# Fused bucket attention and expert layer on one core: one weight chunk more in the attention phase, and small shifts of work between engines

## The reference

```python
q_bits = (einsum('bhsd,dk->bhsk', q, proj) > 0)      # 6 bits, the same for k
mask = q_bucket[:, :, :, None] == k_bucket[:, :, None, :]
scores = where(mask, q @ k.T / sqrt(64), -1e9)
attn_out = softmax(scores) @ v
x = attn_out.transpose(0, 2, 1, 3).reshape(2, 768, 512)
logits = x @ w_gate                                   # 8 experts
local_gate = sigmoid(x @ w_local)
# along s: e = argmax(logits) if s == 0 or local_gate < 0.5, else the previous row's e
h = maximum(x @ w1[e], 0)                             # 512 -> 1024
out = softmax(logits)[e] * (h @ w2[e])                # 1024 -> 512
```

## Time and profile before

| what | value |
|---|---|
| median of 3 runs | 481.82 us (478.69 to 482.27) |
| the profiled execution: time | 481.82 us |
| the profiled execution: span of the trace | 480.0 us |
| mean granted clock of TensorE | 0.982 |
| busy: PE, POOL, ACT, DVE | 453.1, 337.9, 299.2, 260.7 us |

### The profile page before, as it was taken

The page is one execution under the profiler, slowest core; times in us unless marked ns, Lnnn a source line. Parts: engine busy times, 40 slices in busy tenths (PEclk is TensorE's granted clock), DMA queues, the critical chain, the costliest instruction groups (busy, mean ns, idle before and its releaser), DMA issues.

```text
span 480.0 us, 10919 instructions
## 1 busy us (share of the span) xinstructions
PE 453.1 (94%) x4159; PEld 264.4 (55%) x4159; DVE 260.7 (54%) x381; ACT 299.2 (62%) x283; POOL 337.9 (70%) x191
## 2 busy tenths in 40 slices
PE   6879999999999999999988899999999979899994
PEld 3456777777766776777763444444444434344441
DVE  6765667656666666665278488343344324334331
ACT  2358988888889898887886067475566759400000
POOL 1227889898988899999873897678576959951101
PEclk9999999999999999999996999999999989999998
DMA  9654744566555733229739999999999999583440
GB/s 200 169 152 99 211 100 124 155 167 175 145 124 132 260 84 86 54 62 270 96 87 363 270 231 230 218 286 218 237 280 263 265 252 278 114 204 67 88 64 0
DMA packets 156419, 82.54 MB, mean 172 GB/s; under 512 B 101763, under 2 KB 147215, under 8 KB 156370
## 3 DMA queue, kind: packets, MB, share of 16 engines
q1 hardware_dynamic: 108622, 42.49, 41.9%
q10 hardware_dynamic: 44708, 31.22, 26.2%
q0 software_dynamic: 3040, 8.13, 6.0%
HBM read 47.99 MB, written 8.13 MB: 117 GB/s over the span
## 4 chain that ended last, share of the span: by engine, by line
PE 55%; POOL 13%; ACT 11%; ACTq 8%; DVE 4%; DMA 4%; issue 4%; SPq 1%; POOLq 0%; DVEq 0%
POOL W L385 8%; ACTq L1314 7%; PE pA L624 6%; PE pA L625 6%; PE pB L641 6%; PE pB L642 6%; ACT W L1514 5%; PE pO L1461 4%; PE pA L1420 3%; PE pP L1461 3%; PE pO L702 3%; PE pO L699 3%; PE pO L697 3%; DMA room<-room 3%; POOL room L1356 3%
## 5 line engine op out<-in xcount | busy, mean ns | idle before, releaser
L548 POOL TENSOR_TENSOR room<-room 128x1536 f16<-128x1536 f32 x46 | 142.5, 3106 | 35.7 <-ACT room L793 35.6
L897 DVE TENSOR_REDUCE room<-pA 128x2 f32<-128x1536 f32 x46 | 80.8, 1757 | 50.6 <-PE pA L625 50.6
L385 POOL TENSOR_TENSOR W<-room,W 128x1024 f16<-128x1024 f32 x44 | 93.4, 2136 | 20.2 <-ACT W L1514 17.3
L787 ACT ACTIVATE room<-pB 128x1536 f32<-128x1536 f32 x47 | 68.1, 1448 | 35.1 <-PE pB L642 33.8
L793 ACT ACTIVATE room<-room 128x1536 f16<-128x1536 f32 x47 | 69.7, 1484 | 1.5
L697 PE MATMUL pO<-W,room 128*128 128x64 f16 x564 | 60.8, 192 | 0.1
L702 PE MATMUL pO<-W,room 128*128 128x65 f16 x564 | 60.8, 194 | 0.0
L699 PE MATMUL pO<-W,room 128*128 128x65 f16 x564 | 60.7, 193 | 0.0
L641 PE MATMUL pB<-room 128*128 128x512 f16 x192 | 57.9, 326 | 2.0 <-DMA room<-room 1.7
L642 PE MATMUL pB<-room 78*128 78x512 f16 x192 | 57.9, 326 | 0.0
L624 PE MATMUL pA<-room 128*128 128x512 f16 (+1 forms) x184 | 55.4, 326 | 2.3 <-DMA room<-room 2.3
(11 more groups left out here) (226 smaller groups left out, 778.3 us busy)
## 6 DMA issues: line engine op xcount, KB each, us to landing
room<-in_moe_w ACTq DMA_DIRECT2D x44, 256.0 KB, 9.1
room<-room SPq DMA_DIRECT2D x90, 96.0 KB, 2.2
W<-in_moe_w ACTq DMA_DIRECT2D x8, 1024.0 KB, 6.0
XN<-in_moe_w ACTq DMA_DIRECT2D x28, 256.0 KB, 9.4
W<-in_moe_w SPq DMA_DIRECT2D x4, 1024.0 KB, 6.7
room<-in_q SPq DMA_DIRECT2D x16, 192.0 KB, 3.4
W<-in_v ACTq DMA_DIRECT2D x4, 768.0 KB, 5.7
x_rows<-XN SPq DMA_DIRECT2D x12, 256.0 KB, 3.0
```

The lines of the kernel that those rows point to most:

```text
L385: pool.tensor_tensor(parts(r)[:, 1, cols], scaled(r)[:, cols], parts(r)[:, 0, cols], ALU.subtract).then_inc(lows(r, half)[0], 1)
L548: pool.tensor_tensor(PTL[:, n % NP, :, :], E32[:, n % 2, :, :], PTH[:, n % NP, :, :], ALU.subtract).then_inc(s_lo, 1)
L897: dve.reduce_max(RM[:, g % 2, 2 * p:2 * p + 2], scores_in(n)[:, :].rearrange("p (i s) -> p i s", i=2), AX.X).then_inc(s_rmax, 1)
```

## The change

`EARLY` goes from 6 to 7: chunk 6 is done in the attention phase. Its four ACT pieces fall into steps 39 to 42, its two POOL halves both into step 43. The low part of step 44 goes from POOL to DVE (`LAST`). After the attention phase ACT and POOL do chunk 7, and POOL's later list is chunks 8 and 9. One of the 12 row matrices goes from DVE to POOL (`NV`). `FIRST` is 5, with 4 gathers between halves and 6 behind them. The 22 idle matmuls become 17. The two FULL buffers swap places in `STAGES`, because chunk 11 is now in the other one. The issue of the quarters of chunk 14 stands at chunk 11 and not 10. `place_q_low` is written out where it was called, with the same two instructions.

```diff
-        EARLY = NH // 2 - 2
+        EARLY = NH // 2 - 1
...
-        LAST = (NS - 2, NS - 1)
+        LAST = (NS - 4, NS - 2, NS - 1)
...
-                place_q_low(sp, g)
+                sp.wait_ge(s_t2, 2 * g + 2)
+                sp.dma_start(QA[D:P, b, :], T2[0:D, t, :]).then_inc(s_asm[b], 16)
...
-                if 0 <= r < EARLY and u >= 3:
+                if 0 <= r < EARLY - 1 and u >= 3:
                     low_weights(pool, r, u - 3)
+                if r == EARLY - 1 and u == W_STEPS - 1:
+                    low_weights(pool, r, 0)
+                    low_weights(pool, r, 1)
...
-        NV = NC - 2
+        NV = NC - 3
...
-                  + [FULL[:, i, :] for i in range(2)])
+                  + [FULL[:, i, :] for i in (1, 0)])
...
-            FIRST = 6
+            FIRST = 5
...
-            for t in itertools.islice(turn, 3):
+            for t in itertools.islice(turn, 6):
                 gather(t)
...
-            idle_turns(22)
+            idle_turns(17)
```

More of the change, by code:

```diff
@@ L425, in place_k @@
             eng.dma_start(KB[0:D, b, :], T2[D:P, t, :]).then_inc(s_asm[b], 16)
-        def place_q_low(eng, g):
-            eng.wait_ge(s_t2, 2 * g + 2)
-            eng.dma_start(QA[D:P, g % NQ, :], T2[0:D, g % 2, :]).then_inc(s_asm[g % NQ], 16)
         block = ctx.enter_context(nc.Block())
```

## The result

The change makes the kernel slower. 20 executions of the changed kernel have a median of 485.47 us (478.7 to 489.16), 20 of the kernel before beside them 480.62 us (476.49 to 486.51). The ratio is 1.0069, with a 95% interval of 1.0041 to 1.0097, so some 3.3 us are lost; the medians themselves are 4.9 us apart.

A forecast was written before the change was run, and what follows sets the result against it. PE was taken to bound the kernel, losing 5.8 us to streamed-weight waits and low clock. Removing these and starting 0.8 later cut the 480.0 us span to 475.0; with 1.8 around it 476.8, forecast 477.0, range 474.5 to 481.5.

The forecast's parts named there:

- part 2: POOL in attention steps 43 to 45: losing one low part and gaining two weight halves ends the phase 0.7 us later.
- part 4: 17 idle matmuls for 22 ahead of tile 0: PE's stand grows to 2.0 us, the clock holds, cost 0.
- part 6: One chunk fewer between routing and stream: the weight stream is 5.0 us earlier at expert 7, bounds 0 and 5.6.
- the shift of 0.8: PE's start in the expert phase: 0.7 us from the attention phase plus 0.1 from the row matrices, 0.8 later.
- a forecast of 5.8 us: PE in the expert phase: 4.1 us of waits for line 385 plus 1.7 of low clock, all to go.
- rival C: The clock falls in the longer stand ahead of tile 0, PE is 1.7 us later: 478.5 us; chance 0.17.
- Argument (c): Transfers: ACT's queue has 1.5 MB of room at 290 to 300 us, so the earlier stream's 1.1 MB fits.
- rivals B and D: Stream gains only part, 478.3 to 479.8 us, chance 0.20; head start given back whole, 482.6 to 484.3 us, chance 0.08.
- Parts 1, 3 and 5: ACT's chunk 6 pieces in steps 39 to 42, cost 0; row matrices moved, +0.1 us; FIRST = 5, cost 0.

The follow-up runs named there:

- b_again: The kernel before, unchanged, run again for a second profile: 480.62 us, ratio 0.9946 to the session's kernel before.
- b_again2: The kernel before, unchanged, run once more for a third profile: 483.88 us, ratio 1.0001.
- b_idle17: The kernel before with 17 idle matmuls for 22 and nothing else: 482.41 us, ratio 0.9989.
- a_idle22: The changed kernel with 22 idle matmuls instead of 17: 481.65 us, ratio to before 1.0111.
- a_again: The changed kernel, unchanged, run again: 484.12 us, ratio to before 1.0135.
- a_late15: The changed kernel with ACT waiting for tile 0's first down product before the streamed chunks: 485.20 us, ratio to before 1.0136.
- a_halves45: The changed kernel with 22 idle matmuls and POOL's two halves of chunk 6 behind step 45's low part: 486.88 us, ratio to before 1.0049.
- v2: The changed kernel with attention-phase chunks three steps earlier, step 44's low part on POOL, ten row matrices on DVE, 22 idle matmuls: 485.32 us, ratio to before 1.0015.
- b_gap7: The kernel before with chunk 7's POOL halves right behind chunk 6's, ahead of the routing, one chunk fewer behind it: 485.01 us, ratio 1.0127.

## Why the prediction was wrong

The forecast was a gain of 4.8 us and the runs show a loss of 3.3, so 8.1 us have to be accounted for. The two halves on POOL are 1.5 of them (part 2), the clock is 1.3 by an estimate (part 4), and the rest, some 5, is the gain of part 6, of which the times show next to nothing. The first is shown by experiment. The second is shown in the windows and its price is an estimate. The third is what is left over: the runs show that the gain was taken back by other waits, and not what makes these waits long.

**What bounds the kernel** was read rightly, and so was the mechanism of part 6: the waits for line 385 fell from 4.1 to 0.5, the low clock at 387 went, ACT's first line 1504 came at 289.15 (I said 287.8) and chunk 12's low half at 292.49 (292.6, though the terms of the prediction give 291.8; the shift of 0.8 seems to be in it twice). One profile showed this, and the two rows carried a forecast of 5.8 us. What I did not see in one profile is that PE has another wait of the same size at the same transfers: b_again and b_again2, the same kernel, stand 4.4 and 4.7 us for turned rows, where the earlier trace rows has none. Their profiled executions took 484.21 and 488.75 us, the one of the earlier trace rows 481.82, so a quicker execution can be free of that wait.

**Part 2, +0.7 with a bound of +2.4, measured +2.15. The step that failed first.** POOL "gets two weight halves of 2.13 less an overlap, 4.2 us": they took 5.76. The step took prices from rows in which the other engine had no instruction with two inputs beside them, and asked of DVE's low part only whether it might be "slower beside a busy POOL", not whether POOL would be slower beside it. 1.56 us more for the pair and the 0.7 that I had make 2.26. The trace of before had a hint that I passed over: ahead of the pair of line 385 at 292.10 (2.36 us), DVE has another at 284.60 that took 3.31. The second collision, DVE's 3.70 us, cost nothing: its next row starts 1.72 us behind line 802, as it did behind line 801. The third, DVE's halves of chunk 11 beside POOL's of chunk 12, came with the gain of part 6, which had no term for it.

The Trainium skill (SBUF — State Buffer, section "SBUF: two separate sides") states this rule: DVE, when its instruction has two inputs in SBUF, and GpSimd, when its own reads SBUF, share a pair of ports, and the one that starts first holds them for its whole instruction. The runs agree: 0.08 us decided who waited, a pair of 4.22 became 5.76, and 0.26 became 2.07. It was the rule that spoke against this change, and the prediction weighed another one.

**Part 4, cost 0, by the runs some 1.3.** This was rival C, to which I gave 0.17. I chose between a row with 1.18 of 2 us busy, where the clock held, and a stand of 2.8 where it fell, and put 2.0 with the first. It belonged with the second, in four of five profiles. My estimate is 1.6 us, the mean of the four, x 0.8 = 1.3 us. The row of 387 alone told what a fall costs, and of the earlier trace rows I should have seen that the five matmuls were what kept the stand at 0.91.

**Part 6, 5.0 us, by the times next to nothing. The largest term that failed.** Argument (c) said that 1.5 MB of room lay at 290 to 300 by the count of ACT's bytes. The bytes of one queue were the wrong measure. They did not say how long an issue can hold ACT there: it took 7 to 11 us in the five, where the earlier trace rows had 3.4 as the longest of ACT's stands, and the kernel before itself has issues of 7.85 and 9.50 in b_again and b_again2. That SP's transposes and POOL's gathers, which are in flight in that stretch too, fill the room was argued and is not shown. Against PE's own start, which is later, the head start is 5.3 us at chunk 12 and 2.3 at chunk 13, on the means of the two groups. The waits for line 385 fall by 3.8 on the mean (from 4.4 to 0.6, the five against the four in the table), those for turned rows rise by 1.3 (from 2.3 to 3.6). Of the executions that were profiled the quick ones agree: before (481.82 us) and b_idle17 (479.15) have none of these, after (479.41) and a_idle22 (478.45) have 1.7 and 1.8. Where one such wait was 3.8 us or more (b_again2, a_again, a_late15, a_halves45, v2, b_gap7), the clock was at 0.50 for 2 to 5 us behind it, which comes on top. I named in (c) the condition, "if gathers and transposes leave it the room", and gave it no price; rivals B and D had part of it.

How much of the head start is real stays open. 5.0 us are not: with them a_idle22 would be at 2.15 - 5.0 = -2.85 us, 0.994, and its interval begins at 1.0052, further off than the half per cent by which the kernel before differs from itself. b_gap7, whose routing is 2 us longer, lies above with its whole interval too, and v2 (1.6 - 5.0, so 0.993, against 0.9975 and more) fits that but would not be enough alone. By the mean waits it would be 3.8 - 1.3 = 2.5 us, less the clock behind the longer ones. By the stretch from tile 0's first product to the end of the span it would be 3.5, as this is 209.9 us on the mean of the five (206.7 to 213.2) and 213.5 of the four (209.1 to 219.9), a scatter as large as what is looked for. By the ratio of after, 3.3 = 2.15 + 1.3 - x, it is next to nothing, and by the medians, 4.9 us apart, less than that. From step 38's exponentials to the end the five profiles even take 1.2 us less than the four, on the mean: single profiles don't carry the net loss, which is known from the times of many executions alone. What holds up the turned rows in some executions of the same kernel and not in others is not settled: the gathers in a row mostly go with a long issue on ACT, but b_again and b_again2 had one of 7.85 and 9.50 without them.

**Parts 1, 3 and 5** cost what I said, as far as rows show: against step 38's exponentials, those of step 40 are 0.1 us late, of steps 42 and 44 0.4, and those of steps 45 and 46 on time; PE waits 0.3 us for POOL's third row matrix in a_again; and the first half behind FIRST starts where DVE's product lets it.

## What to carry to other kernels

Before work is moved to an engine that shares a port with another, put both timelines side by side with the changed order and look for two instructions that read SBUF at the same time; a short one that meets a long one waits until the long one is done, and the first to start wins. Do this for every place that the change moves, also for those that only come earlier. Matmuls that nobody reads are cover for the clock: count the stand that is left when some are taken away, and price it by the worse of two rows. And when one wait for transfers is removed, ask which other wait hangs on the same transfers, in more than one profile of the same kernel.

## What the runs showed that I had not expected

- A 128 x 96 product on DVE takes 0.26 us alone and 2.07 us beside one half of 2.12 us on POOL; the cost is not that of its own size.
- The clock can fall after a stand of 2.0 us between two busy stretches and is then at 1.2 GHz for some 3 us in which PE is busy for nearly all of it; with such a stand (2.07 us) it held in one of five profiles, and with one of 2.3 us in the attention phase in two of seven.
- One issue of a 256 KB load on ACT's queue took 11.29 us in a_again, and ACT stood 9.49 us for it; one of a transpose took 8.98 us on SP's queue in the kernel after (4.78 before).
